# TensorE's second stage without its loop, three loads for w3's first block, and batch 0's exponent moved ahead of a split

## The reference

```python
scores = scale * x @ state.T ;  a  = softmax(scores)  ; xread = a @ state      # tokens read the states
scores2 = scale * state @ x.T ; a2 = softmax(scores2) ; sread = a2 @ x         # states read the tokens
x = concat([xread, sread], axis=2)      # 8 * (512 + 32) = 4352 rows of 512
h = ((x @ w1) * (x @ w2)) @ w3          # 512 -> 1024 -> 1024
x = h @ w_out                           # 1024 -> 512
h = x @ w_in ; g = h - tanh(h)          # 512 -> 2048   (second stage)
out = g @ w_out2                        # 2048 -> 512
```

## Time and profile before

| what | value |
| --- | --- |
| median of 3 runs | 1253.36 us (1252.82 to 1256.39) |
| the profiled execution's own time | 1250.26 us |
| its span | 1248.5 us |
| PE busy | 1236.2 us, 99% |
| DVE, ACT busy | 800.8 us (64%), 548.5 us (44%) |
| mean granted TensorE clock | 0.999 |
| DMA, slices 1 and 2 of 40 | 371 and 372 GB/s |
| DMA, mean of the span | 51 GB/s |
| queue q8 (instructions) | 58 packets, 0.95 MB |
| queue q14 (instructions) | 22 packets, 0.18 MB |

### The profile page before, as it was taken

The page is one execution under the profiler, slowest core; times in us unless marked ns, Lnnn a source line. Parts: engine busy times, 40 slices in busy tenths (PEclk is TensorE's granted clock), DMA queues, the critical chain, the costliest instruction groups (busy, mean ns, idle before and its releaser), DMA issues.

```text
span 1248.5 us, 17100 instructions
## 1 busy us (share of the span) xinstructions
PE 1236.2 (99%) x6628; PEld 1002.8 (80%) x6628; DVE 800.8 (64%) x1295; ACT 548.5 (44%) x1028; POOL 1.3 (0%) x7
## 2 busy tenths in 40 slices
PE   8999999999999999999999999999999999999998
PEld 6789777777777778888888888878888878888887
DVE  5666566555455335887676676675776666766776
ACT  5663334333333334555344344444344444444444
POOL 0000000000000000000000000000000000000000
PEclk9999999999999999999999999999999999999999
DMA  9932000000000120311101001001001001010000
GB/s 371 372 153 74 12 34 9 27 34 1 34 35 1 68 104 16 102 56 38 43 18 51 1 18 51 1 19 51 1 17 51 9 11 51 18 43 1 10 34 18
DMA packets 17648, 64.05 MB, mean 51 GB/s; under 512 B 1968, under 2 KB 3376, under 8 KB 12960
## 3 DMA queue, kind: packets, MB, share of 16 engines
q1 hardware_dynamic: 16832, 62.00, 13.6%
q10 hardware_dynamic: 704, 0.85, 0.2%
q0 software_dynamic: 32, 0.07, 0.0%
HBM read 45.09 MB, written 17.83 MB: 50 GB/s over the span
## 4 chain that ended last, share of the span: by engine, by line
issue 100%; POOLq 0%; POOL 0%
POOLq L261 0%; POOL ident L439 0%; POOL ident L437 0%; POOLq L439 0%; POOLq L1474 0%
## 5 line engine op out<-in xcount | busy, mean ns | idle before, releaser
L1261 ACT ACTIVATE hq<-bank 128x512 f32<-128x512 f32 (+1 forms) x144 | 82.8, 575 | 398.8 <-PE bank L1387 398.8
L1332 DVE TENSOR_TENSOR hw<-hw,hq 128x512 f32<-128x512 f32 (+1 forms) x144 | 95.5, 663 | 198.5 <-ACT hw L1272 198.4
L1387 PE MATMUL bank<-ysp_hi,wi_lo 128*128 128x512 f32 (+1 forms) x576 | 217.5, 378 | 4.2 <-issue 4.2
L1387 PE MATMUL bank<-ysp_hi,wi_hi 128*128 128x512 f32 (+1 forms) x576 | 217.6, 378 | 0.0
L1387 PE MATMUL bank<-ysp_lo,wi_hi 128*128 128x512 f32 (+1 forms) x576 | 217.3, 377 | 0.0
L1414 PE MATMUL wide<-wz_hi,gsp_hi 128*128 128x512 f32 x544 | 212.3, 390 | 0.3 <-DVE gsp_lo L1322 0.3
L1414 PE MATMUL wide<-wz_lo,gsp_hi 128*128 128x512 f32 x544 | 211.8, 389 | 0.0
L1414 PE MATMUL wide<-wz_hi,gsp_lo 128*128 128x512 f32 x544 | 211.7, 389 | 0.0
L1387 PEld LDWEIGHTS bank<-ysp_hi,wi_lo 128*128 128x128 f32 x576 | 108.3, 188 | 24.9 <-issue 5.0
L1387 PEld LDWEIGHTS bank<-ysp_hi,wi_hi 128*128 128x128 f32 x576 | 108.2, 188 | 21.7 <-DVE gb L1351 1.0
L1387 PEld LDWEIGHTS bank<-ysp_lo,wi_hi 128*128 128x128 f32 x576 | 108.3, 188 | 20.4
(11 more groups left out here) (122 smaller groups left out, 1737.6 us busy)
## 6 DMA issues: line engine op xcount, KB each, us to landing
xT<-in_x_cols SPq DMA_DIRECT2D x8, 1024.0 KB, 9.2
xs<-in_x_rows SPq DMA_DIRECT2D x8, 1024.0 KB, 8.0
y_dram<-ysb SPq DMA_DIRECT2D x8, 1024.0 KB, 3.9
out<-ysb SPq DMA_DIRECT2D x8, 1024.0 KB, 4.6
yr<-y_dram SPq DMA_DIRECT2D x28, 256.0 KB, 4.1
w_raw<-in_moe_w SPq DMA_DIRECT2D x8, 512.0 KB, 10.4
wi_raw<-in_moe_w_in SPq DMA_DIRECT2D x4, 1024.0 KB, 7.2
raw<-in_moe_w_out SPq DMA_DIRECT2D x16, 256.0 KB, 2.6
```

The source lines that it names most:

```text
L1261: act.activation(hq[:, f % 2, 0:w], ph[f % 2][:, 0:w], ACT.Square).then_inc(sq_done, 1)
L1332: dve.tensor_tensor(u, u, q, ALU.mult).then_inc(w2_done, 1)
L1387: mm = pe.matmul(ph[f % 2][:, 0:w], wi[s][c][:, f * P:(f + 1) * P], ysp[k][u][c][:, 0:w], start=c + m == 0, stop=c == KC - 1 and m == LAST)
```

## The change

Four edits.

1. TensorE's loop over tiles 2 to 7 of the second MoE stage becomes a Python loop, so that the code is written out. The loops of ScalarE, VectorE and SyncE stay.
2. w3's block 0 comes in three loads, parts k = 0-1, 2-3 and 4-7, and is split in these three; TensorE's piece n = 1 waits for the second part, pieces 2 and 3 for the third.
3. On SyncE's queue, w_out's second load (k = 2, 3) stands ahead of the third of these loads. ScalarE and VectorE split the third part between w_out's blocks 3 and 4.
4. On ScalarE, `exp_a2(0)` stands ahead of `split_w3(2)`. VectorE's and TensorE's order stay.

```diff
-    FIRST = (slice(0, 2), slice(2, NF1))
+    PARTS = ((slice(0, 2), slice(2, 4), slice(4, NF1)), (slice(0, 2), slice(2, NF1)))
...
         def load_first(n):
-            sp.dma_start(w3r[0][:, FIRST[n], :], w3_cols[0, :, FIRST[n], :]).then_inc(first_in[n], 16)
+            sp.dma_start(w3r[0][:, PARTS[0][n], :], w3_cols[0, :, PARTS[0][n], :]).then_inc(first_in[n], 16)
         for n in range(2):
             load_first(n)
-        for n in range(1, len(WO_LOADS)):
+        load_wo(sp, 1)
+        load_first(2)
+        for n in range(2, len(WO_LOADS)):
             load_wo(sp, n)
         load_w3(sp, 1)
...
     # scalar (vector has the same edit of the order of the splits)
         split_part(0, 1)
-        for k in range(2, NF1):
+        for k in range(2, 4):
+            split_wo(k)
+        split_part(0, 2)
+        for k in range(4, NF1):
             split_wo(k)
         for n in range(2):
             split_part(1, n)
         empty_prod(0)
         copy_st(0)
+        exp_a2(0)
         split_w3(2)
-        exp_a2(0)
...
     # tensor, piece(r, n)
             if r < 2:
-                pe.wait_ge(w3_lo, 2 * r + min(n, 1) + 1)
+                pe.wait_ge(w3_lo, 3 * r + min(n, 2 - r) + 1)
             if n == 0:
                 if r >= 2:
-                    pe.wait_ge(w3_lo, r + 3)
+                    pe.wait_ge(w3_lo, r + 4)
...
     # tensor, second MoE stage
         tile(0, 0)
         tile(1, 1)
-        with pe.Fori(1, PAIRS) as i:
+        for i in range(1, PAIRS):
             tile(2 * i, 0)
             tile(2 * i + 1, 1)
         last_tile(B, 0)
```

More of the change, by code:

```diff
@@ L353, in stage_front @@
     w3_in, w3_hi, w3_lo = [sem(f"w3_in{n}") for n in range(2)], sem("w3_hi"), sem("w3_lo")
-    first_in = [sem(f"first_in{n}") for n in range(2)]
+    first_in = [sem(f"first_in{n}") for n in range(3)]
     STATES = (slice(0, 1), slice(1, 2), slice(2, B))
@@ L444, in split_part @@
             act.wait_ge(first_in[n] if r == 0 else w3_in[1], 16)
-            act.activation(w3T[0][r][:, FIRST[n], :], w3r[r][:, FIRST[n], :], ACT.Copy).then_inc(w3_hi, 1)
+            act.activation(w3T[0][r][:, PARTS[r][n], :], w3r[r][:, PARTS[r][n], :], ACT.Copy).then_inc(w3_hi, 1)
         def split_w3(r):
@@ L566, in split_part @@
         def split_part(r, n):
-            dve.wait_ge(w3_hi, 2 * r + n + 1)
-            dve.tensor_tensor(w3T[1][r][:, FIRST[n], :], w3r[r][:, FIRST[n], :], plain(w3T[0][r][:, FIRST[n], :]), ALU.subtract
+            dve.wait_ge(w3_hi, 3 * r + n + 1)
+            part = PARTS[r][n]
+            dve.tensor_tensor(w3T[1][r][:, part, :], w3r[r][:, part, :], plain(w3T[0][r][:, part, :]), ALU.subtract
                               ).then_inc(w3_lo, 1)
         def split_w3(r):
-            dve.wait_ge(w3_hi, r + 3)
+            dve.wait_ge(w3_hi, r + 4)
             dve.tensor_tensor(w3T[1][r % 2][:, :, :], w3r[r % 2][:, :, :], plain(w3T[0][r % 2][:, :, :]), ALU.subtract
```

## The result

The changed kernel runs at 1245.76 us (median of 4 runs, 1244.92 to 1246.71), the kernel before, in the runs beside it, at 1253.13 (1252.82 to 1256.39). The ratio is 0.9936, 95% interval 0.9917 to 0.9954. The sign and the pauses were forecast, the size was not: off the 1253.36 of before the ratio gives 1245.3, just under the range's lower end of 1245.5 (the median itself, 1245.76, lies just inside), and against the 5.55 us forecast the difference is 7.4 to 8.0.

A forecast was written before the change was run, and what follows sets the result against it. TensorE, busy 1236.2 of 1248.5 us, was taken as the bound, so only its pauses could be won. Gains of 4.91 (loop), 0.13 (loads) and 0.51 (exponent) sum to 5.55, off the median 1253.36: 1247.8 us, range 1245.5 to 1250.8.

The forecast's parts named there:

- 5.55 us: Whole forecast gain: 4.91 from TensorE's loop, 0.13 from edits 2 and 3, 0.51 from edit 4.
- The median of the runs is 3.1 us higher, 1253.36; taken off it: Last step of the sum: the 5.55 us gain subtracted from the runs' median 1253.36, giving 1247.8 us.
- 4.91 us: Extra time of tiles 4 and 6 behind the loop's backward jumps, 2.48 + 2.43, all forecast to go.
- The pause and its cause: At tiles 4 and 6 TensorE runs dry after the jump until the loop's first instructions are fetched again; about 2.3 us.
- a pause that moves or stays: Two rivals: pause moves to ScalarE or VectorE, gain 3.1, chance 0.06; jump isn't the cause, gain 0.64, chance 0.05.
- code that isn't fed: Rival: written-out tiles 2 to 7 pause for about 21 fetches, losing 51 us, time 1299; chance 0.03.
- 0.13 us: Front, edits 2 and 3: w_out's block 4 product starts 0.24 us sooner, less about 0.1 for a second TensorE stop.
- 1.86: Front: product with w_out's block 2 forecast at 8.82 us, with block 4 at 10.68.
- 0.51 us: Front, edit 4: batch 1's scores 0.81 us sooner, less 0.30 lost at w3's block 2.
- The low value named for the front, 0.2 us: Batch 7's columns land at 67.4, scores start at 67.57; if transfers came no sooner, only 0.2 of 0.64 stays.
- these loads are issued on TensorE's own progress and behind one another, and move forward with it: Argument for charging the front nothing for late columns of batch 7, despite 0.2 us of room.
- The first rival: Only the loop pays: transfers or edits 2 and 3 eat the front's gain; gain 4.9, time 1248.5, chance 0.22.

The follow-up runs named there:

- e2: The changed kernel with TensorE's loop put back, so edits 2, 3 and 4 without edit 1: 1252.18 us, ratio 0.9998 to the kernel before.
- e12: The changed kernel with all four edits, measured a third time, on one chip with edit 1 alone: 1244.59 us (1244.46 to 1245.71).
- e11: Edit 1 alone on the kernel before, measured again on the chip of the changed kernel's third measurement: 1244.8 us (1244.62 to 1245.64).
- e4: Edits 2 and 3 alone on the kernel before, loop kept: 1253.03 us, ratio 1.0004.
- e14: Edit 1 alone plus a wait on thirteen GpSimd writes stopping TensorE at the start of tiles 4 and 6: 1257.15 us (1254.06 to 1258.61).
- e5: The changed kernel itself, measured again beside other experiments: 1244.36 us (5 runs), ratio 0.9936 to the kernel before.

## Why the prediction was wrong

- **The step that failed** is in the sum: "The median of the runs is 3.1 us higher, 1253.36; taken off it". It took the 3.1 us between the profiled execution and the median as something the change would leave alone. It was largely the jumps' own cost. The profiled execution was a rare one, with short stops and with half clock behind neither: of 29 runs in one job four were under 1251 us. The term mis-sized is "4.91 us": right for that execution, and between medians 7.6 us on one chip (1252.39 before, 1244.8 with edit 1 alone) and 6.65 on another. What was left out has two parts, the half clock (1.7 us for each stretch of 3.4 us) and a further cost of some 1.6 us that executions at a mean clock of 1.000 show too; how the median divides between them is open. The prediction has the clock only as 1.00 between 22 and 839 us and never asks what it does after a break. The sign to read was at hand: runs from 1252.82 to 1256.39, all above the profiled one.
- **The pause and its cause** were right: the branch, 4.9 us between the first two profiles, no cost at the loop's entry or exit, nothing new late on ScalarE and VectorE. That the pause is the fetch fits q8's three packets; no run sets the fetch apart from the branch. The rivals of a pause that moves or stays, and of code that isn't fed, are out: tiles of 87.04 us.
- **The clock and the branch.** Half clock came behind stops of 2.47 us and more from matmul to matmul, not behind each of them, and behind none of 1.8. The Trainium skill's "TensorE: Matmul & The Clock Gate", section "HAM oscillation — how this bites in real kernels", says that idle gaps throttle the array again, and was the page to weigh. The runs agree, though the waits of the page's example, some 3 to 5 us, are longer than the 2.07 us of idle time behind which it came in e2's profile. A jump's idle time was 1.97 to 2.65 us in the profiles. The 108 ns in the Trainium skill's "Advanced Engine Details and Errata", section "Control Flow Timing", is not the cost of such a jump.
- **Edits 2 and 3.** 0.13 us was forecast and can't be seen in the first profile. Block 4's product started at 10.93 against 10.92, and 1.80 us behind block 2's where 1.86 was worked out; the shift of the whole front by what landed when (w_out's first pair was split from 5.38 instead of 5.04) is larger than the term. Two later profiles, with that split at 4.85 (e12) and 4.86 (e11, edit 1 alone), can be compared: block 4's product started at 10.52 and 10.75, batch 0's scores at 14.81 and 14.92. That is 0.23 and 0.11 us sooner, where 0.24 and 0.13 were forecast: the step was right, and too small to count.
- **Edit 4.** 0.51 us was about right in the place (0.52 at w3's block 2 for all three front edits, of which batch 0's scores, at 15.23 instead of 15.09, had lost 0.14 before) and did not reach the end. The low value named for the front, 0.2 us, for batch 7's columns, was the one to take. "these loads are issued on TensorE's own progress and behind one another, and move forward with it" was wrong as an argument for their landing: those of batch 6, issued at 50.68 in the profile of the changed kernel and at 50.50 in e12, landed 10.7 and 8.4 us later.
- **The first rival**, only the loop pays, had the right mechanism as far as the runs can tell; its 4.9 had the same fault as the forecast's.

## What to carry to other kernels

A stop of TensorE has two prices, the stop and the clock behind it, and a single profile may show only the first. Before a sum is made against one execution, compare its time and clock with the other runs': if it is the fastest of them, what the others have more may belong to the very thing that is being removed. A gain ahead of a bandwidth-bound run of transfers is only worth the room that the tightest of them has, in the execution in which it lands late.

## What the runs showed of the hardware

- Idle times of TensorE at full stream, twice in an execution: with 1.8 us from matmul to matmul never half clock (6 runs), with 2.5 to 2.6 a loss of 1.6 us or more in ten of 11 (in one of the ten at a mean clock of 1.000), with 3.9 in ten of ten. Behind a stop the clock was at 1.2 GHz for some 3.4 us, behind e4's first jump and around the end of e14's second stop for 6.8, while 512-column matmuls start 0.425 us apart. Behind e14's second stop, in the stretch view:

```profile
1022.00:1028.00 6.00, 5.85 (x14) 4.59 (x15) 0.00 (x0) 0.32 (x1) 0.10 (x1) 0.51 0.00 0
```

- A taken backward jump on TensorE over two tiles of code (some 1536 weight loads and matmuls) cost 2.4 to 3.0 us between matmuls in six profiles, in that of before with three instruction packets fetched in 8 us. ScalarE's and VectorE's shorter loops jumped in the same profile without a fetch.
- Loads of 1 MB, issued at the same place, landed up to 3.2 us apart from one execution to the next (7.5 us behind the issue in e5, 10.7 in the first profile), and in one execution stopped TensorE for 1.57 us where two other executions of the changed kernel show no wait at that place.
